# A chunked recurrence: loads on ScalarE's queue, fewer and larger block transfers, and seven slots prepared ahead

## What is computed

```
for t in range(S):                                 # S = 768, state is [B, H, 40, 40]
    y[t]  = r[t] . state
    Sa    = state . a[t]
    state = state * w[t] - outer(Sa, b[t]) + outer(v[t], k[t])
x = y as [B, S, 320]
h = relu(x @ w_in);  c = conv3(h);  x = (h * sigmoid(c)) @ w_out
logits = x @ w_gate; per expert e: softmax(causal(q k^T)) v wo[e], weighted by the top-2 gates
```

## Time and profile before

| | us |
|---|---|
| median of 3 runs | 1005.4 (997.03 to 1009.6) |
| profiled execution, its own time | 1008.42 |
| its span, first to last instruction | 1006.5 |
| TensorE busy | 824.0 |
| VectorE busy | 546.5 |
| ScalarE busy | 311.3 |
| GpSimd busy, all in the recurrence but for a few instructions | 265.0 |

### The profile page before, as it was taken

The page is one execution under the profiler, slowest core; times in us unless marked ns, Lnnn a source line. Parts: engine busy times, 40 slices in busy tenths (PEclk is TensorE's granted clock), DMA queues, the critical chain, the costliest instruction groups (busy, mean ns, idle before and its releaser), DMA issues.

```text
span 1006.5 us, 27784 instructions
## 1 busy us (share of the span) xinstructions
PE 824.0 (82%) x11872; PEld 602.0 (60%) x11872; DVE 546.5 (54%) x1209; ACT 311.3 (31%) x739; POOL 265.0 (26%) x550
## 2 busy tenths in 40 slices
PE   2328989797789988759998789998899987899977
PEld 2228888796789878754454554455544545554555
DVE  7765675566667754124445635437454366353464
ACT  3002231132222322112225532225422255312354
POOL 1287876386667876000000000000000000000000
PEclk9998985787878989789999999999999999999999
DMA  5326556455655646323010000100000000000000
GB/s 138 98 66 126 134 123 135 83 129 113 124 125 136 131 89 146 70 75 106 1 40 8 20 14 1 40 0 21 14 7 16 24 8 20 14 1 0 1 21 20
DMA packets 133305, 61.33 MB, mean 61 GB/s; under 512 B 107328, under 2 KB 120256, under 8 KB 133184
## 3 DMA queue, kind: packets, MB, share of 16 engines
q1 hardware_dynamic: 133184, 59.56, 25.0%
HBM read 45.37 MB, written 14.16 MB: 59 GB/s over the span
## 4 chain that ended last, share of the span: by engine, by line
PE 57%; DVE 15%; SPq 7%; ACT 6%; DMA 6%; issue 5%; POOL 5%; DVEq 0%; ACTq 0%
PE ps_all L715 9%; PE ps_all L699 8%; PE ps_all L756 4%; DMA l_by_unit<-l_blocks 4%; PE ps_all L832 3%; PE ps_all L793 3%; ACT probs L892 3%; SPq L440 3%; PE ps_all L811 3%; PE ps_all L709 3%; PE ps_all L823 2%; POOL t_update L285 2%; PE ps_all L702 2%; POOL t_by_unit L287 2%; PE ps_all L743 2%
## 5 line engine op out<-in xcount | busy, mean ns | idle before, releaser
L285 POOL TENSOR_TENSOR t_update<-l_by_unit,t_by_unit 128x126 f32<-128x126 f32 (+17 forms) x264 | 126.8, 480 | 118.6 <-DVE t_by_unit L287 98.7
L287 POOL TENSOR_TENSOR t_by_unit<-t_by_unit,t_update 128x126 f32<-128x126 f32 (+17 forms) x264 | 132.7, 503 | 20.7
L699 PE MATMUL ps_all<-scaled_then_x,inputs_then_w_up 128*128 128x384 f32 x256 | 90.9, 499 | 14.9 <-DMA scaled_then_x<-y_t 9.2
L102 PE MATMUL ps_scan<-decayed_a_and_eye,scaled_then_x 40*128 40x104 f32 x768 | 67.9, 346 | 38.1 <-DVE decayed_a_and_eye L317 38.1
L983 DVE TENSOR_REDUCE minus_max<-ps_all 128x1 f32<-128x128 f32 (+5 forms) x96 | 55.0, 617 | 75.4 <-PE ps_all L797 75.3
L715 PE MATMUL ps_all<-gated,w_down 128*128 128x384 f32 x256 | 91.1, 499 | 0.0
L102 PEld LDWEIGHTS ps_scan<-decayed_a_and_eye,scaled_then_x 40*128 40x128 f32 x768 | 62.9, 252 | 40.1 <-DVE decayed_a_and_eye L317 24.3
L699 PEld LDWEIGHTS ps_all<-scaled_then_x,inputs_then_w_up 128*128 128x128 f32 x256 | 48.8, 194 | 51.4 <-issue 11.2
L858 ACT ACTIVATE h<-ps_all 128x384 f32<-128x384 f32 x64 | 27.9, 490 | 147.9 <-PE ps_all L702 147.9
L715 PEld LDWEIGHTS ps_all<-gated,w_down 128*128 128x128 f32 x256 | 46.0, 189 | 44.6 <-issue 19.1
L793 PE MATMUL ps_all<-k_t,q_t 64*128 64x512 f32 (+3 forms) x256 | 49.7, 488 | 26.0 <-ACT probs L892 22.2
(11 more groups left out here) (115 smaller groups left out, 1523.0 us busy)
## 6 DMA issues: line engine op xcount, KB each, us to landing
inputs_then_w_up<-in_x SPq DMA_DIRECT2D x48, 160.0 KB
l_by_unit<-l_blocks SPq DMA_DIRECT2D x48, 128.0 KB, 3.7
inputs_then_w_up<-in_x SPq DMA_DIRECT2D x48, 81.4 KB
inputs_then_w_up<-in_x SPq DMA_DIRECT2D x48, 80.0 KB
uv_and_ruv<-in_v SPq DMA_DIRECT2D x48, 80.0 KB, 4.2
r_t<-in_r SPq DMA_DIRECT2D x48, 80.0 KB
v_t<-in_vt SPq DMA_DIRECT2D x48, 80.0 KB
y_t<-y_out SPq DMA_DIRECT2D x24, 160.0 KB
```

Source lines behind the costliest of these rows:

```text
L102: last = nc.tensor.matmul(PS[:, o:o + ROWS], weights, AL[c % NK][rows(h), p, :], start=True, stop=True)
L285: return (lambda: eng.tensor_tensor(tmp[:, 0:cols, 0:rest], l[:, s:s + 1, s + 1:BLK].broadcast_to(shape), t[:, 0:cols, s:s + 1].broadcast_ ...
L287: lambda: eng.tensor_tensor(t[:, 0:cols, s + 1:BLK], t[:, 0:cols, s + 1:BLK], tmp[:, 0:cols, 0:rest], ALU.subtract))
L699: nc.tensor.matmul(bank[n][:, 0:HALF], WIN[:, t, cols], XT[:, t, n * HALF:(n + 1) * HALF], start=(t == 0), stop=False)
```

## The change

GA goes from 6 to 7, and every buffer whose number comes from it grows by one. The loads `load_x`, `load_v` and `load_r` leave SyncE's queue for ScalarE's: `load_x` goes between the move of y and `bkn_move`, `load_v` and `load_r` to the end of the slot. `in_x` is loaded in two DMAs instead of six, and r and v^T, laid out side by side on the host, in two instead of four. `l_in` is issued once per pair, in two DMAs of 64 partitions, in the odd slot; `t_out` likewise in two DMAs; `t_in` of the second unit goes behind `l_in`. `eye_move` goes from the end of the slot to just behind the move of y, in the same even slots. `solve_head(j)` for j of 2 and more stands in slot 2j - 4. Pair 0 is solved by VectorE alone (`solve_first`, in slot -3) and pair 1 by GpSimd alone.

```diff
-GA = 6
+GA = 7
...
         def eye_move(j):
             if j >= 2:
-                for x in range(2):
-                    act.wait_ge(m[f"t_out{x}"], 32 * (j - 1))
+                act.wait_ge(m["t_out"], 32 * (j - 1))
             nc.scalar.activation(TS[j % 2][:, :, :], EYE[:, :, :], ACT.Copy).then_inc(m["eye"], 1)
+        def load_x(c):
+            if c >= 2:
+                act.wait_ge(m["prepped"], c - 1)
+            for h in range(2):
+                act.dma_start(INX[c % 2][rows(h), :], in_x[c, h]).then_inc(m[f"inx{c % 2}"], 16)
...
+        def load_r(n):
+            if n >= 3:
+                act.wait_ge(m["out"], n - 2)
+            for h in range(2):
+                act.dma_start(RV[n % 3][rows(h), :, :, :].rearrange("r k p t -> r (k p t)"),
+                              in_rv[n, h].rearrange("r k p t -> r (k p t)")).then_inc(m[f"r{n % 3}"], 16)
...
             if live: move(YS, PY, "y", "y_sb", n, -1.0)
+            if n % 2 == 0 and 2 <= n // 2 + 2 < NPAIR and n >= 0:
+                eye_move(n // 2 + 2)
+            if 2 <= n + GA + 1 < NT: load_x(n + GA + 1)
             if ahead: bkn_move(c)
...
-            if n % 2 == 0 and 2 <= n // 2 + 2 < NPAIR and n >= 0:
-                eye_move(n // 2 + 2)
+            if n == 2 - GA:
+                for k in range(2):
+                    load_v(k)
+                    load_r(k)
+            if 0 <= n and n + 2 < NT:
+                load_v(n + 2)
+                load_r(n + 2)
...
+        def solve_first():
+            dve.wait_ge(m["l_in"], 32)
+            dve.wait_ge(m["eye"], 1)
+            for s in range(BLK - 1):
...
-            if n % 2 == 1 and 0 <= (n + GA - 3) // 2 < NPAIR: solve_head((n + GA - 3) // 2)
+            if n % 2 == 0 and 2 <= (n + GA - 3) // 2 < NPAIR: solve_head((n + GA - 3) // 2)
             if ahead: gm(g)
+            if n == -3: solve_first()
...
-        def l_in(c):
-            j, x = c // 2, c % 2
-            sp.wait_ge(m[f"l_out{x}"], 64 * (j + 1))
+        def l_in(j):
+            for x in range(2):
+                sp.wait_ge(m[f"l_out{x}"], 64 * (j + 1))
...
             for half in range(2):
-                r = slice(half * 64 + x * 32, half * 64 + (x + 1) * 32)
-                sp.dma_start(LU[j % 2][r, :, :], l_dram[c].rearrange("n p s t -> (n p) s t")).then_inc(m[f"l_in{x}"], 16)
+                sp.dma_start(LU[j % 2][half * 64:half * 64 + 64, :, :],
+                             l_dram[2 * j:2 * j + 2].rearrange("x n p s t -> (x n p) s t")).then_inc(m["l_in"], 16)
...
         for n in range(-GA, NT + 1):
             c = n + GA - 1
-            if n >= -1 and n % 2 == 1 and n + 1 < NT:
+            solved = n >= -1 and n % 2 == 1 and n + 1 < NT
+            if solved:
                 t_out((n + 1) // 2)
-                for x in range(2): t_in(n + 1 + x)
-            if 0 <= c < NT: l_out(c)
-            if n + GA + 2 < NT: load_x(n + GA + 2)
-            if 0 <= n and n + 2 < NT: load_v(n + 2)
-            if 0 <= c < NT: l_in(c)
-            if 0 <= n and n + 2 < NT: load_r(n + 2)
+                t_in(n + 1)
+            if 0 <= c < NT:
+                l_out(c)
+                if c % 2 == 1: l_in(c // 2)
+            if solved: t_in(n + 2)
             if n >= 1 and (n - 1) // 2 % 2 == 1: store(n - 1)
```

More of the change, by code:

```diff
@@ L50, in recurrence @@
     UV = [sb(f"uv_and_ruv{n}", [128, 2, P8, ROWS]) for n in range(3)]
-    VT = [sb(f"v_t{n}", [ROWS, P8, C]) for n in range(3)]
-    RT = [sb(f"r_t{n}", [ROWS, P8, C]) for n in range(3)]
+    RV = [sb(f"r_t_and_v_t{n}", [ROWS, 2, P8, C]) for n in range(3)]
+    RT = [RV[n][:, 0, :, :] for n in range(3)]
+    VT = [RV[n][:, 1, :, :] for n in range(3)]
     XS = sb("x_rhs", [128, P8, D])
@@ L348, in y_out @@
                                     two(pf3(n)[:, :, 0:C]), ALU.mult).then_inc(m["yo"], 1)
+        def solve_first():
+            dve.wait_ge(m["l_in"], 32)
+            dve.wait_ge(m["eye"], 1)
+            for s in range(BLK - 1):
+                mult, sub = step(nc.vector, LU[0], TS[0], TMD, s)
+                link(dve, mult())
+                if s < BLK - 2:
+                    link(dve, sub())
+                else:
+                    sub().then_inc(m["solved"], 1)
         def solve_head(j):
-            for x in range(2):
-                dve.wait_ge(m[f"l_in{x}"], 32 * (j + 1))
+            dve.wait_ge(m["l_in"], 32 * (j + 1))
             dve.wait_ge(m["eye"], j + 1)
-            if j >= 1:
-                dve.wait_ge(m["head"], j)
+            dve.wait_ge(m["solved"], 1)
+            if j >= 3:
+                dve.wait_ge(m["head"], j - 2)
             for s in range(HEAD):
@@ L415, in gpsimd @@
         i.then_inc(m["set_pool"], 1)
-        for j in range(NPAIR):
-            pool.wait_ge(m["head"], j + 1)
-            if j >= 1:
+        for j in range(1, NPAIR):
+            if j == 1:
+                pool.wait_ge(m["l_in"], 64)
+                pool.wait_ge(m["eye"], 2)
+            else:
+                pool.wait_ge(m["head"], j - 1)
                 pool.wait_ge(m["solved"], j)
-            for s in range(HEAD, BLK - 1):
+            for s in range(0 if j == 1 else HEAD, BLK - 1):
                 mult, sub = step(nc.gpsimd, LU[j % 2], TS[j % 2], TMP, s)
@@ L499, in store @@
                 sp.dma_start(dst.rearrange("p e t -> e p t"), YO[x][rows(h), :, :]).then_inc(m[f"stored{x}"], 16)
-        for c in range(2):
-            sp.wait_ge(m["set_inx"], c + 1)
-            load_x(c)
+        sp.wait_ge(m["set_inx"], 1)
+        for h in range(2):
+            sp.dma_start(INX[0][rows(h), :], in_x[0, h]).then_inc(m["inx0"], 16)
         sp.wait_ge(m["set_pool"], 1)
@@ L1085, in load_tokens @@
             load_x(sp, y_t, 0, *early_buffers(inputs, scaled)[1:], xt)
[L1087 removed]
+        ctx, first = recurrence(nc, sem, in_x, in_v, in_rv, l_dram, t_dram, y_t, inputs, scaled,
                                 load_weights, load_tokens)
```

59 lines of the change are left out of this document (23 added, 36 removed).

## The result

| | before | after |
|---|---|---|
| median, us | 1004.0 (4 runs, 997.03 to 1009.6) | 1019.74 (4 runs, 1012.64 to 1023.49) |
| profiled execution, its span | 1006.5 | 1014.5 |
| its granted clock, slots 1 to 17 | 0.82 | 0.83 |

The ratio of the times is 1.0122, with an interval of 1.0071 to 1.0173. The forecast was 988 with a range of 968 to 1008: the change went the other way.

What follows compares the result with a forecast made beforehand. The prediction took the recurrence's chain of hand-overs as the bound, with blocks late in head slots. Against 1008.4 us: -16 - 6 - 3 + 5 + 1 + 1 = -18, so 990.4; for a median 988, range 968 to 1008.

Steps and rivals of the forecast that it cites:

- part 4: Seven slots ahead: the prologue costs 5 us (bounds 0 and 10); slot 18, which no longer prepares, wins 3 us.
- step-through: Prologue, followed slot by slot: slot 0 starts at 79 to 80 us and not at 76.6; 5 us charged.
- Part 5: ScalarE's issues of v and r between the moves of u and x: 0.05 us a slot, 1 us for 22 slots.
- Parts 1 and 2: Head slots: the blocks' read goes out earlier, then the identity is late next; 16 us won (8 to 29).
- Part 3: TensorE's clock behind late heads: shorter pauses win back 6 us of slow stretches, between 0 and 15; lower bound -5.
- rival (D): ScalarE's issues land on the chain between u and the next x: slower, 1033 at 4.3 us; chance 0.08.
- Part 6: The rest of SyncE: its odd slot is covered, but barely with a store; costs 1 us in all.
- (B): Live slots: the clock stays up and a pair takes 27.8 us; 973 on the median; chance 0.27.
- (C): Live slots: the blocks stay late, by SyncE or a double transfer landing in 5.2 us; about 1005; chance 0.20.

Runs made afterwards that it cites:

- later_only: The kernel after with the first loads of v and r two slots later and nothing else changed; 1012.13 us, ratio 1.0047 to the kernel before.
- heads_as_before: The kernel after with pairs 0 and 1 solved as in the kernel before, without `solve_first`; 1029.61 us, ratio 1.0152 to the kernel before.
- t_first: The kernel after with `t_out` and first `t_in` of pair 0 ahead of slot -2's write of the blocks; 1014.72 us, ratio 1.0026 to the kernel before.
- unit_reads: The kernel after with the blocks read unit by unit, on a queue without the loads; 1011.67 us, ratio 1.0081 to the kernel before.
- read_first: The kernel before with the read of the blocks put ahead of the loads, still on SyncE; 1011.14 us, ratio 0.9992 to the kernel before.
- no_vr: The kernel after with the loads of v and r left out from unit 3 on; 1014.77 us, ratio 1.0047 to the kernel before.

## Why the prediction was wrong

**The step that failed is part 4, its charge for the prologue:** +5 us, with bounds of 0 and 10, was +17.1. It is the largest single error but not the whole: of the 26 us between the sum (-18) and the spans (+8.0), the prologue is 12.1, the live slots are 11.2 (parts 1, 2, 3, 5 and 6) and the untouched code is 3.2, less 0.5 in the tail. With the prologue right the spans would still have shown -4, a gain but not the one forecast. The step-through ended with the first blocks of slot 0 at 78 to 81 us; they came at 87.8. Four things were wrong or passed over:

- The step-through has `gm` of slot -3 ending at 41. It ended at 45.2, because the scan waited for x behind the first loads of v and r. Part 5 priced ScalarE's issues in the live slots only and passed over the slot 2 - GA, where eight of them stand in a row. Shown by later_only, 4.4 us earlier at slot -3.
- `solve_first` took 22.2 us, the upper of the two values in the text. But I let the added slot of 7.3 us disappear against the heads that VectorE loses. The mask of slot -2 falls at 73.45; the same unit was masked at 66.84 before; so nothing was left to hide the 7.2 us of the added slot. heads_as_before shows that solving pair 0 by heads would not have hidden it either.
- "SyncE issues slot -2's write until 72 before it reaches `t_out`": the order was seen, and charged with 2 us. The write waits for its mask, so `t_out` went at 76.60, 9.3 us after the solve was over. t_first takes 6.3 us off slot 0.
- From `t_out` to the first blocks I took 6.6 us, from the earlier trace rows. It was 11.2 us, since its landing took 7.29. Even with the inverses in time TensorE could not have begun before 84.1 (87.77 less the wait of 3.68), since by then the masks were late: the 78 to 81 were out of reach. And the head placed in slot 0 was priced at its 4.7 us of work, without the wait for its blocks, which was 10.24.

The single shares don't add up exactly, since a wait taken away in one place comes back in part in the next: later_only's head in slot 0 still waits 10.3 us.

**Parts 1 and 2, the heads:** -16 us became -7.6. The read of the blocks does go out right behind the landing of the write. But it landed after 4.7 us, not the 3.7 of the earlier trace rows, and the sentence that "the larger pieces carry two units' bytes at once, but x and v no longer stand ahead" let the two cancel by hope. The runs separate the causes: with both units read at the late time, 4.7 us in two DMAs and 3.9 in four, and the same 6.3 to 6.4 from first issue to last landing; without the traffic of v and r, 4.3; with only one unit's bytes, 2.9 (unit_reads) and 2.5 (read_first). It is mainly the bytes asked for at that moment; the 3.7 us of the earlier trace rows were a unit's read behind loads of x and v still under way. The rule of the Trainium skill cited beside the sum (page "DMA: Bandwidth & Descriptors", section "Issuing engines are not separate DMA queues"), that issuing from several engines saves only issue time, fits: a unit's read ahead of the loads lands as early with them on SyncE's queue (2.5) as with them on ScalarE's (2.9). That the identity is late next was right: three of the eight live heads wait for it, and six in unit_reads.

**Part 3, the clock:** -6 became 0. The granted clock was 0.83 against 0.82. The pauses were shorter, yet `all_blocks` still took 1.93 us behind six of the eight live heads (before: behind five); its fast value is 1.13. Timeline of TensorE after:

```profile
147.20 1.13 PE L174 MATMUL ps_scan<-x_rhs,block_inverse_t 64*64 64x40 f32 x32
...
163.22 1.93 PE L174 MATMUL ps_scan<-x_rhs,block_inverse_t 64*64 64x40 f32 x32 [3.09 <-ACT x_rhs L228]
...
225.60 1.16 PE L174 MATMUL ps_scan<-x_rhs,block_inverse_t 64*64 64x40 f32 x32 [3.60 <-ACT x_rhs L228]
...
256.84 1.93 PE L174 MATMUL ps_scan<-x_rhs,block_inverse_t 64*64 64x40 f32 x32 [4.42 <-ACT x_rhs L228]
```

A pause of 3.09 us is followed by the slow form and a longer one, of 3.60, by nearly the fast one. In the first the granted clock fell to 0.50 inside the pause, at 161.7; in the second it was 1.00 throughout the pause and fell only at 226.6, 1.0 us behind its end; at 256.84 it had been 0.50 since 250.5, before the pause began. So my reading of the earlier trace rows, that the length of the pause sets what follows it, is wrong. What sets it stays open; I ran nothing on it.

**Part 4, slot 18:** -3 was -3.5 over the whole tail. Right.

**Part 5:** +1 was about +6. By the gaps between u_t and x it is 0.26 us a slot in the kernel after (0.39 in its repeat), 6 to 9 us over 22 slots, and no_vr gives it back but for 0.04. This is the mechanism of rival (D) at a third of the 18 us at which I let it decide: the four issues take 2.75 us and not 2.1, since the load that now brings r with v^T takes 0.56 us to issue and not r's 0.33; my point for (D) was 3.0. The sign that I named for (D), a gap of over 2.6 us from the end of u's move to x, could not tell anything: its mean was 2.67 before already, and is 2.94 after.

**Part 6:** +1 for SyncE can't be told apart in the live slots. Its real price was in the prologue.

The four lines of the first table give +17.1 - 8.8 - 3.5 + 3.2 = +8.0 us, the difference of the spans. Within the -8.8, heads (-7.6) and issues (+4.2 for 16 slots) leave -5.4 to which I can't give a place.

**The rivals.** None was it. (B) needed the clock, (C) comes near in the live slots (blocks late by the double transfer), but forecast no change because it had the same +5. The rival on the slower side was put on ScalarE's live issues, while the profile of before already held the better one: the earlier trace rows show a preparation slot of 7.3 us with hardly any wait in it, so that an added one has no slack to go into.

**How sure.** The slowdown was 1.2% in the result and 0.5% by the ratio of the repeat (1.3% by its medians). That the kernel after is not faster is shown by both; the exact size is not. The longer prologue is in every profile: in the nine with seven slots and neither `t_out` nor the first loads of v and r mended, the mask of slot 1 comes at 114.4 to 121.1 us, in the five with six slots at 97.7 to 103.1.

## What to carry to other kernels

A pipeline that prepares one slot further ahead moves a whole slot from the steady state into the fill, where here nothing overlapped it. Step the fill through queue by queue, with the waits that each new entry stands behind, before counting anything won in the loop. A wait removed need not be worth anything by itself: ask what else the same queue brings late, as the reading of the blocks first shows, where 31 us of waits went and the time stayed. And when work is merged or preloaded, look at which queue its first instances sit in: a load that isn't needed for 50 us stood ahead of one that was needed at once.

## What the runs showed of the hardware

- The landing time of the blocks' read followed the bytes asked for together: two DMAs of 128 KB land after 2.5 to 2.9 us (median; 3.7 in the kernel before, behind loads of x and v), two of 256 KB after 4.0 to 5.3. The same bytes in four DMAs land after 3.9 each, but from the first issue to the last landing they take 6.3 us, against 6.4 in two.
- A DMA's issue is dear in either queue: 0.64 us for v, 0.56 for r with v^T and 0.35 for x on ScalarE (medians), and up to 1.8 us in single cases. The engine's next instruction starts only behind it: in 5 of 22 slots x started within 0.05 us of its end.
- The first `t_out`, a write of 256 KB, took 7.0 to 7.9 us from its first issue to its last landing in the eight profiles with a load of x issued within 0.8 us of it and the blocks' write just ahead, and 3.5 to 4.2 us in the seven without; which of the two it shares the time with so dearly was not isolated.
